# Unit-block transposes of the next tile inside a tile's down products, later last ranks, and another engine that waits for the outputs

## The reference

```python
# 1. retention: state = gamma*state + k^T v, y = q state / 8   (4 batches, 8 heads, 768 steps, width 64)
# 2. a dense block over 3072 tokens: h = x @ w_in; g = relu(h) + alpha*min(h, 0); x = g @ w_out   (512 -> 2048 -> 512)
# 3. a mixture of 8 experts, one expert a token:
xn = x / (norm(x) + 1e-6); en = expert_emb / (norm(expert_emb) + 1e-6)
expert_idx = argmax(xn @ en.T / tau); gate_w = softmax(...)[expert_idx]
for e in range(8):
    h = maximum(x[expert_idx == e] @ w1[e], 0)              # w1: 512 x 1024
    out[expert_idx == e] = gate_w[...] * (h @ w2[e])        # w2: 1024 x 512
```

## Time and profile before

| | |
|---|---|
| three runs, median (lowest to highest) | 979.59 us (979.33 to 980.65) |
| the profiled execution's own time | 980.66 us |
| its span, first to last instruction | 978.8 us |
| TensorE busy | 957.6 us (98%) |
| VectorE, ScalarE, GpSimd busy | 579.2, 256.1, 241.9 us |
| mean granted TensorE clock | 0.993 of 2.4 GHz |

### The profile page before, as it was taken

One profiled execution on the slowest core, in us unless ns is written; L12 is line 12 of the kernel. 1 busy time (PEld: TensorE's weight loads), 2 busy tenths in 40 slices (PEclk: granted clock), 3 DMA queues, 4 the chain that ended last, 5 costly groups with the idle time before them and its releaser, 6 DMA issues.

```text
span 978.8 us, 16568 instructions
## 1 busy us (share of the span) xinstructions
PE 957.6 (98%) x5448; PEld 795.9 (81%) x5449; DVE 579.2 (59%) x1079; ACT 256.1 (26%) x405; POOL 241.9 (25%) x192
## 2 busy tenths in 40 slices
PE   8999999999999999999999999999999999999995
PEld 7888888888888888888887888877888888888884
DVE  4656589647964697469855987664342642523541
ACT  4222121112111111111111322332343533423531
POOL 4443123331433143414341224120000110000000
PEclk9999999999999999999999999989999999999998
DMA  8431393032002300140012223346331461523310
GB/s 290 165 130 55 122 375 109 0 112 105 0 0 86 129 0 0 43 150 1 1 44 83 80 85 104 113 154 235 129 130 43 170 245 43 181 71 122 126 44 32
DMA packets 27122, 100.48 MB, mean 103 GB/s; under 512 B 4383, under 2 KB 4767, under 8 KB 22448
## 3 DMA queue, kind: packets, MB, share of 16 engines
q1 hardware_dynamic: 19280, 80.90, 23.2%
q0 software_dynamic: 4336, 12.61, 3.3%
q10 hardware_dynamic: 3456, 6.32, 2.3%
HBM read 87.19 MB, written 24.20 MB: 114 GB/s over the span
## 4 chain that ended last, share of the span: by engine, by line
PE 96%; DVE 1%; DMA 1%; issue 0%; ACT 0%; SPq 0%; POOL 0%; ACTq 0%; POOLq 0%; DVEq 0%
PE bank L676 27%; PE bank L694 27%; PE bank L769 15%; PE bank L801 15%; PE bank L572 2%; PE bank L784 2%; PE bank L618 2%; PE bank L588 2%; PE bank L605 1%; PE bank L661 1%; DMA en_all<-in_qk 1%; DVE attention L877 1%; PE bank L640 0%; PE bank L634 0%; PE bank L648 0%
## 5 line engine op out<-in xcount | busy, mean ns | idle before, releaser
L676 PE MATMUL bank<-activations_split,weights_split 128*128 128x512 f32 x1152 | 277.5, 391 | 0.4 <-issue 0.4
L694 PE MATMUL bank<-weights_split,activations_split 128*128 128x512 f32 x1152 | 276.0, 389 | 0.0
L694 PEld LDWEIGHTS bank<-weights_split,activations_split 128*128 128x128 f32 x1152 | 216.1, 188 | 44.9
L676 PEld LDWEIGHTS bank<-activations_split,weights_split 128*128 128x128 f32 x1152 | 215.1, 188 | 45.8 <-issue 1.5
L1493 POOL TENSOR_TENSOR activations_split<-scratch,activations_split 128x512 fp32r<-128x512 f32 x84 | 116.9, 1391 | 327.0 <-ACT activations_split L1280 319.6
L1280 ACT CAST activations_split<-scratch 128x512 fp32r<-128x512 f32 x96 | 59.8, 622 | 412.1 <-DVE scratch L917 412.1
L769 PE MATMUL bank<-weights_split,activations_split 128*128 (+1 forms) x648 | 157.5, 398 | 0.8 <-DVE activations_split L1121 0.8
L801 PE MATMUL bank<-weights_split,activations_split 128*128 (+1 forms) x648 | 155.0, 394 | 2.3 <-ACT activations_split L1379 1.5
L801 PEld LDWEIGHTS bank<-weights_split,activations_split 128*128 128x128 f32 x648 | 119.6, 188 | 26.9 <-issue 2.9
L769 PEld LDWEIGHTS bank<-weights_split,activations_split 128*128 128x128 f32 x648 | 121.1, 191 | 24.9 <-issue 1.0
L976 DVE SCALAR_TENSOR_TENSOR attention<-rows,en_all 128x512 f32<-128x512 f32 x140 | 135.0, 1005 | 0.0
(11 more groups left out here) (183 smaller groups left out, 680.0 us busy)
## 6 DMA issues: line engine op xcount, KB each, us to landing
attention<-in_w_exp SPq DMA_DIRECT2D x24, 1024.0 KB, 5.2
attention<-in_kv SPq DMA_DIRECT2D x43, 256.0 KB, 3.8
expert_rows<-in_pad_rows SPq DMA_DIRECT2D x8, 1028.0 KB, 18.1
en_all<-in_w_exp SPq DMA_DIRECT2D x8, 1024.0 KB, 7.6
rows<-in_w_mlp SPq DMA_DIRECT2D x14, 512.0 KB, 3.3
rows<-expert_rows ACTq DMA_DIRECT2D x24, 257.0 KB, 2.8
attention<-in_qk SPq DMA_DIRECT2D x12, 512.0 KB, 4.7
scratch<-in_qk SPq DMA_DIRECT2D x10, 512.0 KB, 3.7
```

Source lines behind the costliest of these rows:

```text
L676: last = mm(H_ps[f % 2][:, :], win(a, kc, f), x[:, kc, :], start=(k == 0), stop=(k == 3 * KC - 1))
L694: last = mm(bank[j][:, :], x[f % 2][:, j * P:(j + 1) * P], wout(a, f), start=(f == 0 and a == 0 and part_ == "hi"), stop=(f == FB - 1 and ...
```

## The change

It has four parts.

- `h_transpose(t+1)` leaves the head of TensorE's tile t+1 and stands between the two halves of `expert_down(t)`. VectorE's `h_lo_part(t+1)` and ScalarE's `h_hi_part(t+1)` accordingly move to the end of tile t, behind `w2_part`. The wait of `h_hi_part` on down products is loosened by one tile. Tile 2 is written out by hand.
- The last `router_rank` and the count matmul stand behind `up(1, half 0)` rather than ahead of it. `x_transpose(0, 3)` stands between the halves of `up(2)`.
- Of the conditional tiles, the last one no longer makes the transposes and splits for tiles that don't exist, and the conditions are nested: the first false one leaves them all.
- The waits for the outputs are taken off GpSimd's list and stand at the end of ScalarE's.

```diff
@@ TensorE
             def tile(i, tt, e):
                 t = 4 * i + tt
                 e_next = expert_of(t + 1)
-                h_transpose(t)
                 up(t + 1, tt + 1, 0, e_next)
                 up(t + 1, tt + 1, 1, e_next)
                 x_transpose(i, tt + 2)
-                expert_down(t, tt, e)
+                expert_down(t, tt, e, between=lambda: h_transpose(t + 1))
                 return e_next
...
             up(0, 0, 1, 0, between=last_logits)
+            up(1, 1, 0, 0)
             router_rank(NC - 1)
             mm(CNT_ps, ones, seen[:, :, B], start=True, stop=True).then_inc(s_cnt, 1)
-            up(1, 1, 0, 0)
             h_transpose(0)
             up(1, 1, 1, 0)
...
             up(2, 2, 0, e)
+            x_transpose(0, 3)
             up(2, 2, 1, e)
-            x_transpose(0, 3)
-            for tt in (2, 3):
-                e = tile(0, tt, e)
+            e_next = expert_of(3)
+            up(3, 3, 0, e_next)
+            h_transpose(2)
+            up(3, 3, 1, e_next)
+            x_transpose(1, 0)
+            expert_down(2, 2, e, between=lambda: h_transpose(3))
+            e = tile(0, 3, e_next)
...
+            def next_hidden(t):
+                if t + 1 < TILES:
+                    with pe.If(used > t + 1):
+                        h_transpose(t + 1)
+
             for t in range(SURE, TILES):
                 with pe.If(used > t):
-                    h_transpose(t)
+                    e = expert_of(t)
                     if t + 1 < TILES:
                         with pe.If(used > t + 1):
                             e_next = expert_of(t + 1)
                             up(t + 1, t + 1, 0, e_next)
                             up(t + 1, t + 1, 1, e_next)
-                    if t + 2 < TILES:
-                        x_transpose(t // 4, t % 4 + 2)
-                    expert_down(t, t, expert_of(t))
+                            if t + 2 < TILES:
+                                x_transpose(t // 4, t % 4 + 2)
+                    expert_down(t, t, e, between=lambda: next_hidden(t))
@@ VectorE
             w1_part(next_expert(2))
+            x_lo_part(3, 3)
+            split_expert(1, (2,))
             relu_half(2)
-            x_lo_part(3, 3)
-            split_expert(1, (2, 3))
+            split_expert(1, (3,))
+            h_lo_part(2, 2)
 
             def tile(i, tt, e):
                 t = 4 * i + tt
-                h_lo_part(t, tt)
                 e_next = next_expert(t + 1)
                 w1_part(e_next)
                 relu_half(t + 1)
                 x_lo_part(t + 2, tt + 2)
                 w2_part(e)
+                h_lo_part(t + 1, tt + 1)
                 return e_next
@@ ScalarE
-                    act.wait_ge(s_M2, due(s_M2, t - 1 if isinstance(t, int) and t == 1 else t))
+                    act.wait_ge(s_M2, due(s_M2, t - 1 if not isinstance(t, int) or t else 0))
...
                 if not (isinstance(t, int) and t == 2):
                     load_rows(act, i, tt + 3)
-                h_hi_part(t, tt)
                 e_next = next_expert(t + 1)
                 w1_part(e_next, t)
                 relu_half(t + 1)
                 x_hi_part(t + 2, tt + 2)
                 w2_part(e, t)
+                h_hi_part(t + 1, tt + 1)
                 y_part(t, i, tt)
                 return e_next
...
-            for t in range(SURE, TILES):
+
+            def rest(t):
                 with act.If(used > t):
...
+                    if t + 1 < TILES:
+                        rest(t + 1)
+                    act.wait_ge(s_osc[t % 4], due(s_osc[t % 4], 16 * (t // 4 + 1)))
+
+            rest(SURE)
+            for s in s_osc:
+                act.wait_ge(s, due(s, 16 * (SURE // 4)))
@@ GpSimd
-            for s in s_osc:
-                pool.wait_ge(s, due(s, 16 * (SURE // 4)))
-            for t in range(SURE, TILES):
+            def rest(t):
                 with pool.If(used > t):
                     scatter_tile(t, t)
-                    pool.wait_ge(s_osc[t % 4], due(s_osc[t % 4], 16 * (t // 4 + 1)))
+                    if t + 1 < TILES:
+                        rest(t + 1)
+
+            rest(SURE)
```

More of the change, by code:

```diff
@@ L1236, in _ @@
             used = tiles_used(dve)
-            for t in range(SURE, TILES):
[L1238 to L1245, removed]
+            for t in range(SURE, TILES - 1):
+                with dve.If(used > t + 1):
+                    w1_part(next_expert(t + 1))
+                    relu_half(t + 1)
+                    if t + 2 < TILES:
+                        x_lo_part(t + 2, t + 2)
                     w2_part(next_expert(t))
+                    h_lo_part(t + 1, t + 1)
         @block.scalar
@@ L1415, in _ @@
             x_hi_part(3, 3)
-            act.wait_ge(s_pads, due(s_pads, 16 * E))
+            h_hi_part(2, 2)
             def tile(i, tt, e):
@@ L1427, in tile @@
                 w2_part(e, t)
+                h_hi_part(t + 1, tt + 1)
                 y_part(t, i, tt)
                 return e_next
-            e = next_expert(2)
-            for tt in (2, 3):
-                e = tile(0, tt, e)
+            e = tile(0, 2, next_expert(2))
+            act.wait_ge(s_pads, due(s_pads, 16 * E))
+            e = tile(0, 3, e)
             with act.Fori(1, SURE // 4) as i:
@@ L1443, in _ @@
                         load_rows(act, t // 4, t % 4 + 3)
-                    h_hi_part(t, t)
                     if t + 1 < TILES:
-                        w1_part(next_expert(t + 1), t)
                         with act.If(used > t + 1):
+                            w1_part(next_expert(t + 1), t)
                             relu_half(t + 1)
-                        if t + 2 < TILES:
-                            x_hi_part(t + 2, t + 2)
-                    w2_part(next_expert(t), t)
+                            if t + 2 < TILES:
+                                x_hi_part(t + 2, t + 2)
+                            w2_part(next_expert(t), t)
+                            h_hi_part(t + 1, t + 1)
                     y_part(t, t // 4, t % 4)
```

## The result

| | before | after |
|---|---|---|
| median of 15 runs | 979.92 us (979.07 to 980.79) | 981.91 us (981.55 to 983.71) |
| ratio, 95% interval | | 1.0022 (1.0014 to 1.0029) |
| span of the profiled execution | 978.8 us | 979.9 us |
| mean granted clock in it | 0.993 | 0.998 |
| TensorE busy in it | 957.6 us | 956.0 us |

The changed kernel is 2 us slower. The forecast was 0.4 us faster, inside its range, but with the wrong sign.

The account below looks back on a forecast made before the run. TensorE, busy 96%, was taken as the bound, so only its waits, low clock and the end could count. Terms -3.4 - 0.75 - 1.06 - 2.4 + 7.2 = -0.4 us gave 979.2 us from the median; range 975.3 to 982.6 (8 in 10).

Parts of the forecast that it names:

- Cost 1: Six weight-split tiles: the moved transposes wait for VectorE's relu behind two splits, 1.2 us each, +7.2 us in all.
- Gain 1: Last ranks and tile 0: twelve up(1, half 0) matmuls fill TensorE's wait at full clock, -3.4 us.
- only the wait goes: Bound of the term for the last ranks: the wait goes but the clock still falls, -1.8 us.
- Gain 2: Tile 3: earlier x_transpose(0, 3) removes the wait for its x_lo, -0.75 us (0 to -1.15, with 0.40 of issue).
- Gain 3: Last tile: shorter gap ahead of its down products, with the bank's read-out late next, -1.06 us (0 to -1.9).
- Gain 4: Kernel end: without output waits GpSimd's DRAIN starts at about 971.1 and takes 4.98 us again, -2.4 us.
- No obstacle: Rival: the splits cause waits of only 0.3 us in the six tiles; 5.4 us less, 973.8; chance 0.12.
- Late DRAIN: Rival: GpSimd's DRAIN starts its work only when the outputs have landed; 1.4 us more, 980.6; chance 0.17.
- Clock at the logits: Rival: the clock still falls behind the logits; twelve matmuls and ranks cost about 1.5 us more, 980.7; chance 0.11.
- Clock in the new waits: Rival: the six new mid-tile waits bring TensorE's clock down, say 3 us per fall; 985 with two; chance 0.06.

Follow-up runs that it names:

- e1: Changed kernel with VectorE's relu of up(t+1, half 1) ahead of w1_part's two weight splits instead of behind them; 972.67 us, ratio to before 0.9928.
- e3: Kernel before with only the last ranks and the counts put behind up(1, half 0); 977.31 us, ratio to before 0.9975.
- e7: Kernel before with eight useless matmuls between the last logits and the last ranks, filling TensorE's wait for VectorE; 977.80 us, ratio to before 0.9978.
- e2: Kernel before with only the waits for the outputs taken from GpSimd and put at the end of ScalarE's list; 977.23 us, ratio to before 0.9970.
- e9: Changed kernel with h_transpose(t+1) four matmuls later from tile 2 on; 976.67 us, ratio to before 0.9965.
- e5: Changed kernel with ScalarE reading the next expert's number (a table load) ahead of load_rows, not behind it; 979.28 us, ratio to before 0.9993.

## Why the prediction was wrong

**The mechanism that decides was right, its price was not.** Cost 1 named the six tiles, the relu behind the splits and the place of the wait. Its term was 7.2 us; the profile says 9.0, and taking it away (e1) gains 9.2. The step that failed is "The wait is 0.97 us ... That is 1.2 us in each, 6 x 1.2": the tile of the earlier trace rows stood for all six. The parts, as measured:

| part of cost 1 | forecast | profile |
|---|---|---|
| six waits | 5.8 (0.97 each) | 7.2 (1.08 to 1.11 in four, 1.32 and 1.51 in the two that open a round) |
| starting again behind each | 1.2 (0.2 each) | 1.3 (0.22 each) |
| late `up` behind the tile that closes a round | 0 | 0.4 |

Of the 1.4 us that the waits are longer, 0.9 lies in the two tiles that open a round, where ScalarE's queue has the loop's register work and one more table load on its way to the split. The rest is 0.11 to 0.14 in each of the others; in the tile shown, the relu 0.06 later than forecast (T + 10.10, not T + 10.04), TensorE there 0.02 earlier, and 0.06 from the relu's end to the first transpose. The late `up` is the 1.63 us of the tile shown, with 0.12 in the next, against 1.33 in an ordinary one. Two of the forecast's guesses held: starting again costs the 0.2 that was put for it, and the copies that left ScalarE's path bring the split 0.25 us sooner after T, where 0.3 was put.

**The second step that failed is the way from the profiled execution to the median.** The sum was made against the profiled execution and moved by a constant of 1.07 us. Over 15 runs that execution lies 0.74 above the median of the kernel before, and the changed kernel's lies at its median. So 0.8 us of the gain that the profile shows isn't there at the median. By what is argued under e3 and e7 it belongs to gain 1: in the profile 3.06 (3.27 from the last logits on) against a forecast of 3.4, at the median 2.5 (e3).

**Gain 1** had its mechanism right: the twelve products at full clock in the wait, then a wait for `h_lo(0)` (0.94 us at L801) and the relu from 644.50 where 644.25 was forecast. "VectorE's table chain takes the place of the wait removed" held, and e7 shows the rest of it: nearly all of the gain is the clock. That doesn't fit the forecast's own bound of -1.8 for "only the wait goes", since the wait by itself brought 0.4 (3.25 less 2.88).

**Gain 2** was 1.15, not 0.75: the 0.40 of issue behind VectorE's last operation went as well, the bound that was named and not taken.

**Gain 3** was 0.89 against 1.06. The read-out that is late next costs 0.99 us, not 0.82.

**Gain 4** was right in its mechanism and a little small: 2.8 in the profile, 2.6 at the median (e2). The DRAIN counts from the end of the DMA instruction, 0.3 us sooner than the forecast's start of 971.1. The Trainium skill (VectorE: DVE Perf Modes, section The DRAIN you can't avoid) gives some 12 ns for the DRAINs of a program's preamble and postamble on all five engines. At the block's end the traces of before and after agree for the other engines (7 to 17 ns). For GpSimd they don't: 4.98 to 5.94 us over the runs, and e2 shows that this isn't a wait for the outputs.

**The rivals.** No obstacle: fell (six waits). Late DRAIN: fell (e2). Clock at the logits: fell (1.00 through the ranks). Clock in the new waits: fell; after 1.11 us of idle, the products at 836.47 run at full speed. In the profile the terms of the sum were off by 1.8 (cost 1), 0.3, -0.4, 0.2 and -0.4 us, so the two gains that were put too low made up for part of the rest, which was luck. The 1.5 us that are left turn -0.4 into +1.1, and the 0.8 of the way to the median makes it 2.0. The forecast put 0.21 on slower, mostly by way of rivals. Its outermost bounds of 972 and 986 aren't the sums of its terms' bounds either, which come to 971.1 and 987.8; nothing else hangs on them.

What stays open: where in an execution of the second kind the clock falls, as none of these was profiled; why a wait makes the next `up` late in the tile that closes a round; and what the trimmed conditional tiles win by themselves, as no run has them alone.

## What to carry to other kernels

Moving work nearer to its producer is free only as far as the producer's engine is free: list what stands ahead of it on that engine in the rarest kind of tile too, here six of 27, which lost 9.0 us in the profile where the other parts won 7.9. When a move shortens a distance, move the producer up in its own engine's order in the same edit; here that one swap turned 2 us of loss into 7 of gain. When two terms nearly cancel, price each place where a cost recurs from its own rows (here the tiles that open and close a round of the loop differ from the ordinary ones), and look at whether the profiled execution is a typical one before a difference in it is taken to the median.

## What the runs showed of the hardware

- TensorE's granted clock fell to 1.2 GHz in a wait of 1.77 us behind the last logits (products of 128 x 8 in turn with full ones), 1.2 us into it, and came back behind the twelve full products, which took 5.15 us (before, 634.6 to 641.4). The wait of 1.46 us at the last tile (before) and those of 1.08 to 1.51 us in the six tiles (after) left it at 2.4 GHz. Eight useless products in the wait kept it up and made the kernel 2.3 us faster (e7).
- GpSimd's DRAIN at the block's end ended 4.90 to 4.95 us after the last DMA instruction where it began with or during it (after, e2), and 4.98 us after its own start where the engine had been idle (before), whether the last output had landed when the DRAIN started (before) or not (e2). Taking the waits for outputs off that engine let it start sooner and made the kernel 2.6 us faster.
- Four 128x128 transposes behind a wait took 0.66 us, four in a stream 0.44: a wait cost 0.22 us more than its idle time (after, e9).
- A table load into a register with the work behind it cost ScalarE 0.6 us on the way to its next operation where nothing covered it (0.95 us behind the DMA issue in the changed kernel, 0.35 in e5).
